# A gated feed-forward kernel whose first two iterations leave each unit's result in PSUM, with a reordered head

## The chip, the cores and the metric

The kernel runs on one NeuronCore of a Trainium2 chip. The metric is device time in microseconds (us), the median of the timed executions. The engines are TensorE (PE in the profile), VectorE (DVE), ScalarE (ACT), GpSimd (POOL) and SyncE (SP), which here only issues DMAs.

## The reference

Tokens 8192 (2 x 4096), model width 192, hidden width 2048; all data is fp32.

```python
def _attn_ref(x, weight_gen) -> np.ndarray:
...
    w = np.exp(w)
    w = w / (np.sum(w, axis=-1, keepdims=True) + 1e-09)
    pad = K - 1
    x_pad = np.concatenate([np.zeros((B, pad, D), dtype=np.float32), x], axis=1)
    idx = np.arange(S)[:, None] + np.arange(K)[None, :]
    x_unf = x_pad[:, idx, :]
    x_unf = x_unf.reshape(B, S, K, H, group)
    out = np.einsum('bshk,bskhg->bshg', w, x_unf)
...
def _moe_ref(x, w_in, w_out):
    h = x @ w_in
    g = h * np.cos(h)
    return (g @ w_out).astype(np.float32)
...
def _moe2_ref(x, w_in, w_out):
    h = x @ w_in
    g = np.maximum(0.01 * h, h)
    return (g @ w_out).astype(np.float32)
...
    x = _moe_ref(x=x, **moe_kwargs)
    return _moe2_ref(x=x, **moe2_kwargs)
```

There are 8 heads (`H`) and 7 taps (`K`).

## The kernel before

The tokens are cut into 16 chunks (`C`) of 512 (`N`), four from each of 128 partitions. For each chunk there are three parts: the window attention (`attention`, 11 instructions on VectorE: seven multiplications called taps, and four additions, into `prods`), the first network, and the second. Every fp32 product is made of products of high and low parts (`_hi`, `_lo`), since the matmuls take fp32r.

A network's 2048 hidden columns are eight **units** of two 128-column tiles. A unit goes: TensorE fills a PSUM **slot** (two banks, `slots[step % 3]`, three slots) with h; then VectorE and ScalarE form the gated value; ScalarE rounds it to `g_hi` (`high_part`, line 548), and VectorE subtracts to get `g_lo` (`pending_low`, line 710); then TensorE sums `g_hi` and `g_lo` times the output weights into the banks `acc_a` and `acc_b`. In the first network the gated value takes four instructions: `whole` (ACT, 603), the fraction (DVE, 774), the sine (ACT, 639) and the product (DVE, 788). In the second it is one Prelu (ACT, 607). In both, the result goes to the SBUF buffer `gate`, which has two halves, `q % 2`, as `g_hi` and `g_lo` have.

One **iteration** i has 18 steps. Steps 0 to 7 are units q = 0 to 7 (first network, chunk i). Steps 8, 9, 10, 11, 12, 14, 15, 17 are q = 8 to 15 (second network, chunk i - 1). Step 13 transposes an output (from iteration 2 on) and step 16 the next input, also through a slot; in iteration 0 the input has step 8. Everything is written out by hand: each engine has its own list and waits on counting semaphores. TensorE runs `both_products(i, q, j, r)`: five pairs of matmuls that begin filling unit q's slot, then the sum of unit r = q - 3 mixed with the rest of the filling.

Three rules set the order around the change.

- `wait_for_slot`: before a fill, the slot's last use must be over. Before, that is `g_ready` (a first unit's product is written to `gate`) or `leaky_ready` (its Prelu is).
- `high_part` waits for `summed` up to unit s - 2, because `g_hi` has two halves.
- `step_of` on ScalarE: at each step first the pending `g_hi` of the step before, then the sine, then the first read of the next step's slot (`first_read`: `whole` or Prelu). On VectorE: fraction, pending `g_lo`, product, then attention instructions by the table `ATT_AT` and softmax pieces by `SOFT_START` and `SOFT_END`.

The head (iterations -1 and 0) loads everything, does the softmax of the first chunks, the attention of chunk 0 on VectorE, splits the weights of the first network into high and low parts (ACT high, POOL low), and shares the attention of chunk 1 between VectorE (two taps and the last two additions) and GpSimd (seven instructions in the middle). Meanwhile TensorE runs matmuls without use (`raise_clock`). The weights of the second network are split by GpSimd in iteration 0 and 1.

## Time and profile before

| | us |
|---|---|
| median of 3 timed runs | 1177.25 |
| lowest, highest | 1176.35, 1177.26 |
| the profiled execution, its own time | 1180.46 |
| its span, first to last instruction | 1178.7 |
| TensorE busy in it | 1151.8 (98%) |
| VectorE, ScalarE, GpSimd busy | 905.8, 738.6, 94.8 |

TensorE is busy nearly throughout, so the time is the matmuls' own, plus the stretches in which TensorE waits, plus what a lowered clock costs. The chain that ended last is 90% TensorE.

### The profile page before, as it was taken

Reading aid. Unit: us, or ns where it says so; the run is one execution under the profiler, and the core shown is the slowest. Engines: PE = TensorE matmul, PEld = TensorE weight load, DVE = VectorE, ACT = ScalarE, POOL = GpSimd, SP = SyncE. Lnnn points to the kernel's source line nnn. Section 1 sums busy time; section 2 is a strip of 40 time slices with the busy share of each in tenths; the row PEclk is TensorE's granted clock in tenths of the full one; section 3 lists DMA queues with packets and bytes.
Section 4 is the critical chain, followed back from the end, with each engine's and each line's share of the span. In section 5 each row is a group of like instructions: output and inputs, shape, how many; then the busy total and the mean of one; then the engine's idle time right before and its main releaser. Section 6 shows DMA issues by size and latency. Waiting matters only on the chain.

```text
span 1178.7 us, 23306 instructions
## 1 busy us (share of the span) xinstructions
PE 1151.8 (98%) x10180; PEld 960.2 (81%) x10180; DVE 905.8 (77%) x857; ACT 738.6 (63%) x809; POOL 94.8 (8%) x87
## 2 busy tenths in 40 slices
PE   7879999999999999999999999999999999999998
PEld 5658888887878888888888888888888888888876
DVE  7778798787987869688686978868698786968533
ACT  5657675766847657575665756557575665757544
POOL 4764000000000000000000000000000000000000
PEclk9879999999999999999999999999999999999999
DMA  9400101001010010100001010010101001000000
GB/s 268 144 2 1 34 1 37 12 1 48 1 46 3 1 48 2 48 1 17 32 2 48 2 48 1 1 48 1 48 1 48 2 1 48 1 14 1 9 7 28
DMA packets 15277, 32.68 MB, mean 28 GB/s; under 512 B 5068, under 2 KB 9546, under 8 KB 14920
## 3 DMA queue, kind: packets, MB, share of 16 engines
q1 hardware_dynamic: 15176, 31.19, 8.4%
q8 instruction: 81, 1.33, 0.5%
q14 instruction: 20, 0.16, 0.0%
HBM read 24.89 MB, written 6.29 MB: 26 GB/s over the span
## 4 chain that ended last, share of the span: by engine, by line
PE 90%; DVE 4%; ACT 2%; POOL 2%; issue 1%; ACTq 0%; DVEq 0%; POOLq 0%
PE slot L940 41%; PE acc_a L940 27%; PE acc_b L940 18%; DVE g_lo L710 1%; PE slot L1136 1%; POOL prods L282 1%; DVE gate L774 1%; POOL prods L288 1%; PE acc_b L913 0%; DVE prods L282 0%; PE slot L885 0%; ACT gate L607 0%; ACT L656 0%; ACT whole L603 0%; PE slot L872 0%
## 5 line engine op out<-in xcount | busy, mean ns | idle before, releaser
L940 PE MATMUL acc_a<-g_hi,out_hi_lo 64*128 64x512 f32 x2000 | 698.9, 389 | 0.0
L710 DVE TENSOR_TENSOR g_lo<-gate,g_hi 128x1024 fp32r<-128x1024 f32 x256 | 319.7, 1249 | 115.8 <-ACT g_hi L548 115.2
L940 PEld LDWEIGHTS acc_a<-g_hi,out_hi_lo 64*128 64x128 f32 x2000 | 369.6, 185 | 36.0
L940 PE MATMUL acc_b<-g_hi,out_hi_lo 64*128 64x512 f32 x1000 | 389.8, 390 | 8.9 <-DVE g_lo L710 7.5
L940 PE MATMUL acc_a<-g_lo,out_hi_lo 64*128 64x512 f32 x1000 | 388.1, 388 | 0.0
L940 PE MATMUL acc_b<-g_lo,out_hi_lo 64*128 64x512 f32 x1000 | 387.8, 388 | 0.0
L548 ACT ACTIVATE g_hi<-gate 128x1024 fp32r<-128x1024 f32 x256 | 271.4, 1060 | 104.4 <-PE acc_b L940 82.9
L940 PE MATMUL slot<-x_a_hi,in_a_lo 64*128 64x512 f32 x1024 | 300.8, 395 | 1.6 <-DVE gate L788 1.3
L940 PE MATMUL slot<-x_a_hi,in_a_hi 64*128 64x512 f32 x1024 | 297.2, 388 | 0.0
L940 PE MATMUL slot<-x_a_lo,in_a_hi 64*128 64x512 f32 x1024 | 297.1, 388 | 0.0
L940 PE MATMUL slot<-x_b,in_b_hi 64*128 64x512 f32 x1024 | 296.9, 387 | 0.2 <-DVE x_b L724 0.2
L607 ACT ACTIVATE gate<-slot 128x1024 f32<-128x1024 f32 x128 | 130.9, 1023 | 130.0 <-PE slot L940 94.9
L940 PEld LDWEIGHTS acc_b<-g_hi,out_hi_lo 64*128 64x128 f32 x1000 | 184.8, 185 | 33.8 <-DVE g_lo L710 9.8
L940 PEld LDWEIGHTS acc_a<-g_lo,out_hi_lo 64*128 64x128 f32 x1000 | 185.0, 185 | 17.8
L940 PEld LDWEIGHTS acc_b<-g_lo,out_hi_lo 64*128 64x128 f32 x1000 | 185.0, 185 | 16.4
L774 DVE SCALAR_TENSOR_TENSOR gate<-slot,whole 128x1024 f32<-128x1024 f32 x128 | 156.2, 1220 | 50.3 <-ACT whole L603 49.6
L603 ACT ACTIVATE whole<-slot 128x1024 int32<-128x1024 f32 x128 | 131.0, 1023 | 69.3 <-PE slot L940 69.3
L788 DVE SCALAR_TENSOR_TENSOR gate<-slot,gate 128x1024 f32<-128x1024 f32 x128 | 156.4, 1222 | 6.7 <-ACT gate L639 5.0
L940 PEld LDWEIGHTS slot<-x_a_hi,in_a_lo 64*128 64x128 f32 x1024 | 143.0, 185 | 22.5 <-PE slot L940 2.9
L639 ACT ACTIVATE gate<-gate 128x1024 f32<-128x1024 f32 x128 | 135.5, 1058 | 35.8 <-DVE gate L774 33.2
L940 PEld LDWEIGHTS slot<-x_b,in_b_hi 64*128 64x128 f32 x1024 | 142.5, 185 | 18.9 <-DVE x_b L724 0.5
L940 PEld LDWEIGHTS slot<-x_a_lo,in_a_hi 64*128 64x128 f32 x1024 | 142.5, 185 | 18.6 <-DVE x_a_lo L721 0.2
(87 smaller groups left out, 1058.0 us busy)
## 6 DMA issues: line engine op xcount, KB each, us to landing
x_win<-in_x SPq DMA_DIRECT2D x14, 960.0 KB, 4.7
out<-result SPq DMA_DIRECT2D x16, 384.0 KB, 2.4
out_raw<-in_moe_w_out SPq DMA_DIRECT2D x2, 1024.0 KB, 14.1
taps_w<-in_weight_gen SPq DMA_DIRECT2D x2, 560.0 KB, 8.2
out_raw<-in_moe_w_out SPq DMA_DIRECT2D x2, 512.0 KB, 11.0
in_a_raw<-in_moe_w_in SPq DMA_DIRECT2D x1, 1024.0 KB, 9.0
in_b_raw<-in_moe_w_in SPq DMA_DIRECT2D x2, 512.0 KB, 10.8
in_a_raw<-in_moe_w_in SPq DMA_DIRECT2D x2, 384.0 KB, 6.3
```

The lines of the kernel that those rows point to most:

```text
L282: engine.tensor_tensor(prods[:, to, :].rearrange("p (r g) -> p r g", g=group), view[:, k * heads:(k + J) * heads, :], w.unsqueeze(2).to_br ...
L288: engine.tensor_tensor(prods[:, to, :], prods[:, a, :], prods[:, b, :], ALU.add).then_inc(att, 1)
L548: nc.scalar.activation(g_hi[:, q % 2, :], gate[:, q % 2, :], ACT.Copy)\
L603: nc.scalar.activation(whole[:, q % 2, :], slot, ACT.Identity, bias=0.25)\
L607: nc.scalar.activation(gate[:, q % 2, :], slot, ACT.Prelu, alpha=0.01)\
L639: nc.scalar.activation(gate[:, q % 2, :], gate[:, q % 2, :], ACT.Sin, scale=TURN).then_inc(cos_ready, 1)
L710: nc.vector.tensor_tensor(g_lo[:, q % 2, :], gate[:, q % 2, :], g_hi[:, q % 2, :].bitcast(FP32), ALU.subtract)\
L774: nc.vector.scalar_tensor_tensor(gate[:, q % 2, :], slot, 0.25, whole[:, q % 2, :], ALU.add, ALU.subtract)\
L788: nc.vector.scalar_tensor_tensor(gate[:, q % 2, :], slot, RADIANS, gate[:, q % 2, :], ALU.mult, ALU.mult)\
L940: return nc.tensor.matmul(to, w[rows, :], x[rows, :], start=start, stop=stop)
L1136: nc.tensor.matmul(slots[LAG - 1][:, 0, :], g_hi[:, 0, N + k % 2 * P:N + (k % 2 + 1) * P], g_hi[:, 0, 0:N], start=True, stop=True)
```

## The change

Four things are changed together.

1. **Results stay in the slots** in iterations 0 and 1 (`stays`, `result_of`): the product or the Prelu is written back over the slot, and `g_hi` and `g_lo` are made from the slot instead of `gate`. `wait_for_slot` then waits for `lo_ready` of the slot's unit in place of `g_ready` or `leaky_ready`.
2. **The first unit in halves**: unit 0's six steps between fill and sum are twelve instructions of 512 columns, with semaphores `unit_act` and `unit_dve`.
3. **The head**: softmax chunks are (0,1), (1,3), ... in place of (0,2), (2,3), ...; the softmax product of the second and the two VectorE taps of chunk 1 move behind units 1, 2 and 3; the output weights of the first network load in two halves and ahead of chunk 1's window; ScalarE makes their high parts one step later; GpSimd does two taps of chunk 1 between the first and the second piece of their low parts; the last two additions of chunk 1 come after step 6, not 5 (`ATT_END`); at step 7 the split of the next input comes behind the pending `g_hi` and `g_lo`.
4. **Later softmax pieces** are moved: the three exponentials (two table loads each) from (1,13), (2,16), (3,16) to (1,10), (3,10), (5,10), and their beginnings and ends with them.

```diff
+    def stays(i):
+
+
+        return i <= 1
...
-        ATT_DVE, ATT_POOL, ATT_END = 2, 9, 5
+        ATT_DVE, ATT_POOL, ATT_END = 2, 9, 6
...
-        SOFT_CHUNKS = [(0, 2), (2, 3), (3, 6), (6, 11), (11, C)]
+        SOFT_CHUNKS = [(0, 1), (1, 3), (3, 6), (6, 11), (11, C)]
...
-        SOFT_START, EXP_AT, SOFT_END = [[(1, 9), (2, 14), (3, 14)], [(1, 13), (2, 16), (3, 16)],
-                                        [(1, 15), (3, 9), (4, 9)]]
+        SOFT_START, EXP_AT, SOFT_END = [[(1, 8), (2, 13), (4, 13)], [(1, 10), (3, 10), (5, 10)],
+                                        [(1, 13), (3, 13), (5, 13)]]
...
+        def result_of(i, q):
+
+            if stays(i):
+                return slots[UNITS[q] % SLOTS][:, :, :].rearrange("p a n -> p (a n)")
+            return gate[:, q % 2, :]
...
+            load_gen(0)
+            load_own(0)
+            load_halo(0)
+            load_columns(0)
+            load_gen(1)
+            load_columns(1)
+            load_columns(2)
+            load_out(W1, w_out1, slice(0, TILES // 2), out_loaded[0])
+            load_out(W1, w_out1, slice(TILES // 2, TILES), out_loaded[1])
+            load_own(1)
+            load_halo(1)
...
+            for n in range(len(LO_PIECES)):
+                column_lows(n)
+            out_lows(0)
...
-            pool.wait_ge(att, ATT_STEPS + ATT_DVE)
-            for instruction in list(attention(1, pool))[ATT_DVE:ATT_POOL]:
+            of_pool = list(attention(1, pool))[ATT_DVE:ATT_POOL]
+            for instruction in of_pool[:2]:
+                instruction()
+            for n in range(1, len(OUT_PIECES)):
+                out_lows(n)
+            for instruction in of_pool[2:]:
                 instruction()
...
             def high_part(i, q):
                 s = unit(i, q)
+                if s == 0:
+                    act.wait_ge(unit_dve, 2)
+                    nc.scalar.activation(g_hi[:, 0, 0:N], slots[0][:, 0, :], ACT.Copy)\
+                        .then_inc(unit_act, 1)
+                    act.wait_ge(g_ready, 1)
+                    nc.scalar.activation(g_hi[:, 0, N:], slots[0][:, 1, :], ACT.Copy)\
+                        .then_inc(hi_ready, 1)
+                    return
...
-                nc.scalar.activation(g_hi[:, q % 2, :], gate[:, q % 2, :], ACT.Copy)\
+                nc.scalar.activation(g_hi[:, q % 2, :], result_of(i, q), ACT.Copy)\
                     .then_inc(hi_ready, 1)
...
-                    nc.scalar.activation(gate[:, q % 2, :], slot, ACT.Prelu, alpha=0.01)\
+                    nc.scalar.activation(result_of(i, q), slot, ACT.Prelu, alpha=0.01)\
                         .then_inc(leaky_ready, 1)
...
-                    nc.vector.tensor_tensor(g_lo[:, q % 2, :], gate[:, q % 2, :],
+                    nc.vector.tensor_tensor(g_lo[:, q % 2, :], result_of(i - b, q),
                                             g_hi[:, q % 2, :].bitcast(FP32), ALU.subtract)\
                         .then_inc(lo_ready, 1)
...
-                    nc.vector.scalar_tensor_tensor(gate[:, q % 2, :], slot, RADIANS,
+                    nc.vector.scalar_tensor_tensor(result_of(i, q), slot, RADIANS,
                                                    gate[:, q % 2, :], ALU.mult, ALU.mult)\
                         .then_inc(g_ready, 1)
...
-            softmax_end(1)
-
-            first_two = list(attention(1, dve))
-            first_two[0]()
+            softmax_inverse_sum(1)
+
+            of_chunk_1 = list(attention(1, dve))
             for step in range(STEPS):
                 step_of(0, step)
-                if 0 < step < ATT_DVE:
-                    first_two[step]()
+                if step == 1:
+                    softmax_multiply(1)
+                if 1 < step <= ATT_DVE + 1:
+                    of_chunk_1[step - 2]()
                 if step == ATT_END:
-                    for instruction in first_two[ATT_POOL:]:
+                    for instruction in of_chunk_1[ATT_POOL:]:
                         instruction()
...
                 j, s = used[-1]
                 what = kind(j, s)
-                if what == "first":
+                if what in ("first", "second") and stays(j):
+                    if unit(j, UNITS.index(s)) == 0:
+                        pe.wait_ge(unit_dve, 3)
+                    pe.wait_ge(lo_ready, unit(j, UNITS.index(s)) + 1)
+                elif what == "first":
                     pe.wait_ge(g_ready, first_units(j, UNITS.index(s)))
                 elif what == "second":
                     pe.wait_ge(leaky_ready, second_units(j, UNITS.index(s)))
```

How the instructions stand, at three places. In these rows `slot0` to `slot2` are the three slots and `[waits ...]` names the semaphores that an instruction waits for.

TensorE, iteration 1: the first matmul that fills unit 13 (step 14), unit 14 (step 15), unit 15 (step 17), and unit 0 of iteration 2. Before:

```order
L940 MATMUL slot2<-x2_a_hi,in2_a_lo 128x512 [waits leaky_ready]
...
L940 MATMUL slot0<-x2_a_hi,in2_a_lo 128x512 [waits leaky_ready]
...
L940 MATMUL acc_a<-g_hi,out2_hi_lo 128x512 [waits att,leaky_ready]
...
L940 MATMUL slot0<-x1_a_hi,in1_a_lo 128x512 [waits x1_hi,leaky_ready]
```

Now (the same places in the list; the third is the wait ahead of the input transposes):

```order
L1055 MATMUL slot2<-x2_a_hi,in2_a_lo 128x512 [waits lo_ready]
...
L1055 MATMUL slot0<-x2_a_hi,in2_a_lo 128x512 [waits lo_ready]
...
L1055 MATMUL acc_a<-g_hi,out2_hi_lo 128x512 [waits att,lo_ready]
...
L1055 MATMUL slot0<-x1_a_hi,in1_a_lo 128x512 [waits x1_hi,lo_ready]
```

What moved is the semaphore, from the Prelu of the slot's unit to its `g_lo`; the matmuls stand as they stood.

ScalarE, iteration 1, from the Prelu of unit 11 to the Prelu of unit 14. Before (the first row is unit 11's Prelu):

```order
L607 ACTIVATE gate<-slot2 128x1024 [waits lo_ready,filled]
L548 ACTIVATE g_hi<-gate 128x1024 [waits summed,leaky_ready]
L607 ACTIVATE gate<-slot0 128x1024 [waits lo_ready,filled]
L548 ACTIVATE g_hi<-gate 128x1024 [waits summed,leaky_ready] x2
L607 ACTIVATE gate<-slot2 128x1024 [waits lo_ready,filled]
L661 ACT_TABLE_LOAD
L661 ACTIVATE taps_w<-taps_w 128x672 [waits soft]
L656 ACT_TABLE_LOAD
L656 ACTIVATE spare<-ident 1x1
L607 ACTIVATE gate<-slot0 128x1024 [waits lo_ready,filled]
```

Now:

```order
L671 ACTIVATE slot2<-slot2 128x1024 [waits lo_ready,filled]
L732 ACT_TABLE_LOAD
L732 ACTIVATE taps_w<-taps_w 128x672 [waits soft]
L727 ACT_TABLE_LOAD
L727 ACTIVATE spare<-ident 1x1
L607 ACTIVATE g_hi<-slot1 128x1024 [waits summed,leaky_ready]
L671 ACTIVATE slot0<-slot0 128x1024 [waits lo_ready,filled]
L607 ACTIVATE g_hi<-slot2 128x1024 [waits summed,leaky_ready]
L607 ACTIVATE g_hi<-slot0 128x1024 [waits summed,leaky_ready]
L671 ACTIVATE slot2<-slot2 128x1024 [waits lo_ready,filled]
L671 ACTIVATE slot0<-slot0 128x1024 [waits lo_ready,filled]
```

The exponential with its two table loads moved from behind unit 13's Prelu to ahead of unit 10's `g_hi`.

GpSimd in the head: the low parts of the output weights (`out1_hi_lo`, four pieces of two instructions) and its share of chunk 1's attention (`prods`). Before, from the last piece on:

```order
L484 TENSOR_TENSOR out1_hi_lo<-out1_raw,out1_hi_lo 128x4x64 [waits w1_hi]
L484 TENSOR_TENSOR out1_hi_lo<-out1_raw,out1_hi_lo 128x4x128
L282 TENSOR_TENSOR prods<-x_win1,taps_w 128x768 [waits att]
L282 TENSOR_TENSOR prods<-x_win1,taps_w 128x768
L288 TENSOR_TENSOR prods<-prods 128x1536 [waits att]
```

Now, from the second instruction of the first piece to the end of the second:

```order
L525 TENSOR_TENSOR out1_hi_lo<-out1_raw,out1_hi_lo 128x4x128
L297 TENSOR_TENSOR prods<-x_win1,taps_w 128x768 [waits filled,x_zeroed,att,halo1_loaded,own1_loaded,soft]
L297 TENSOR_TENSOR prods<-x_win1,taps_w 128x768
L525 TENSOR_TENSOR out1_hi_lo<-out1_raw,out1_hi_lo 128x4x64 [waits w1_out_hi]
L525 TENSOR_TENSOR out1_hi_lo<-out1_raw,out1_hi_lo 128x4x128
```

Two of the taps moved from behind the fourth piece to behind the first.

## Rows read from the trace of the kernel before

**Rows 1.** The page: busy time of each engine, and one group of instructions.

```profile
PE 1151.8 (98%) x10180; PEld 960.2 (81%) x10180; DVE 905.8 (77%) x857; ACT 738.6 (63%) x809; POOL 94.8 (8%) x87
...
L788 DVE SCALAR_TENSOR_TENSOR gate<-slot,gate 128x1024 f32<-128x1024 f32 x128 | 156.4, 1222 | 6.7 <-ACT gate L639 5.0
```

**Rows 2.** Timeline of PE: start, duration, instruction, count, idle before and releaser.

```profile
34.78 0.79 PE L940 MATMUL acc_b<-g_hi,out_hi_lo 64*128 64x512 f32 x1 [2.19 <-DVE g_lo L710]
...
63.14 0.37 PE L872 MATMUL slot<-ident,prods 64*128 64x64 f32 x2 [4.86 <-DVE prods L288]
...
65.31 0.80 PE L913 MATMUL acc_b<-g_hi,out_hi_lo 128*128 128x512 f32 x1 [1.06 <-DVE g_lo L710]
...
85.60 0.79 PE L940 MATMUL acc_b<-g_hi,out_hi_lo 64*128 64x512 f32 x1 [2.50 <-DVE g_lo L710]
```

**Rows 3.** Windows: stretch, length, five engines' busy time, clock, DMA share, GB/s.

```profile
28.00:32.00 4.00, 2.68 (x22) 1.57 (x22) 2.87 (x3) 3.20 (x5) 2.76 (x4) 1.00 0.99 230
...
64.00:68.00 4.00, 2.94 (x12) 2.16 (x8) 3.32 (x5) 3.79 (x6) 0.00 (x0) 0.50 0.02 6
68.00:72.00 4.00, 4.00 (x17) 2.73 (x17) 3.97 (x4) 1.89 (x2) 1.03 (x1) 0.56 0.00 0
...
84.00:88.00 4.00, 2.40 (x12) 1.91 (x14) 4.00 (x4) 1.58 (x3) 3.92 (x5) 0.65 0.01 4
```

**Rows 4.** Timeline of POOL in the head.

```profile
41.38 2.00 POOL L484 TENSOR_TENSOR out_hi_lo<-out_raw,out_hi_lo 128x256 fp32r<-128x256 f32 x2 [3.38 <-ACT out_hi_lo L686]
43.34 4.04 POOL L282 TENSOR_TENSOR prods<-x_win,taps_w 128x768 f32<-128x768 f32 x2
47.45 4.39 POOL L288 TENSOR_TENSOR prods<-prods 128x1536 f32<-128x1536 f32 x1
...
55.92 3.47 POOL L288 TENSOR_TENSOR prods<-prods 128x1536 f32<-128x1536 f32 x1
59.47 1.54 POOL L282 TENSOR_TENSOR prods<-x_win,taps_w 128x768 f32<-128x768 f32 x1
```

**Rows 5.** Timeline of DVE, iteration 1.

```profile
82.37 3.18 DVE L710 TENSOR_TENSOR g_lo<-gate,g_hi 128x1024 fp32r<-128x1024 f32 x1
...
124.81 1.75 DVE L288 TENSOR_TENSOR prods<-prods 128x1536 f32<-128x1536 f32 x1
126.59 0.96 DVE L282 TENSOR_TENSOR prods<-x_win,taps_w 128x768 f32<-128x768 f32 x1
127.47 1.22 DVE L710 TENSOR_TENSOR g_lo<-gate,g_hi 128x1024 fp32r<-128x1024 f32 x1
```

**Rows 6.** Timeline of PE, first matmuls of units 12, 14, 15 and of iteration 2.

```profile
124.81 0.40 PE L940 MATMUL slot<-x_a_hi,in_a_lo 64*128 64x512 f32 x2
...
133.43 0.39 PE L940 MATMUL slot<-x_a_hi,in_a_lo 64*128 64x512 f32 x2
...
138.18 0.47 PE L940 MATMUL slot<-x_a_hi,in_a_lo 64*128 64x512 f32 x2
...
142.62 0.39 PE L940 MATMUL slot<-x_a_hi,in_a_lo 64*128 64x512 f32 x2
```

**Rows 7.** Timeline of ACT, iteration 1, steps 10 to 16.

```profile
124.98 1.03 ACT L607 ACTIVATE gate<-slot 128x1024 f32<-128x1024 f32 x1 [1.90 <-DVE g_lo L710]
...
133.70 1.07 ACT L548 ACTIVATE g_hi<-gate 128x1024 fp32r<-128x1024 f32 x1 [2.94 <-PE acc_b L940]
...
135.69 1.28 ACT L661 ACT_TABLE_LOAD   x1
...
139.17 1.00 ACT L607 ACTIVATE gate<-slot 128x1024 f32<-128x1024 f32 x1
140.08 0.57 ACT L560 ACTIVATE x_a_hi<-slot 128x512 fp32r<-128x512 f32 x1
...
141.81 2.13 ACT L548 ACTIVATE g_hi<-gate 128x1024 fp32r<-128x1024 f32 x2
```

**Rows 8.** Waits of PE from 160 to 1100 us: us, times, longest.

```profile
PE acc_b L940 <- DVE g_lo L710: 2.5, 2, 1.3
PE acc_b L940 <- DVE res_b L745: 1.4, 2, 0.7
```

More of the change, by code:

```diff
@@ L222, in window_attention_two_ffn @@
         in_loaded = [sem(f"in{n}_loaded") for n in range(3)]
-        out_loaded = sem("out_loaded")
+        out_loaded = [sem(f"out{n}_loaded") for n in range(2)]
         w2_loaded = [sem(f"w2_{n}_loaded") for n in ("a", "b", "out")]
@@ L309, in rest_of_window, with third, start @@
                     engine.wait_ge(halo_loaded[c], 64)
+            def third():
+                if c == 1:
+                    wait_for_chunk()
+                    wait_for_halo()
+                tap(4, 2)
+            def start():
+                wait_for_chunk()
+                tap(6, 0)
+            def rest_of_window():
+                wait_for_halo()
                 tap(5, 1)
@@ L599, in first_read @@
                 slot = slots[step % SLOTS][:, :, :].rearrange("p a n -> p (a n)")
+                if unit(i, q) == 0:
+                    for cols, done in ((slice(0, N), unit_act), (slice(N, None), whole_ready)):
+                        nc.scalar.activation(whole[:, 0, cols], slot[:, cols], ACT.Identity, bias=0.25)\
+                            .then_inc(done, 1)
+                    return
                 if step in FIRST_UNITS:
@@ new lines, in column_turns, with column_highs_b @@
+            def column_turns(n):
+                cols = HI_PIECES[n]
+                a_raw = W1.in_a_raw[:, cols]
+                nc.scalar.activation(a_raw, a_raw, ACT.Copy, scale=PER_TURN).then_inc(w1_hi, 1)
+                nc.scalar.activation(b_lows(W1.in_b_lo_raw, cols), b_pairs(W1.in_b_raw, cols), ACT.Copy,
+                                     scale=PER_TURN).then_inc(w1_raw, 1)
+            def column_highs_b(n):
+                cols = HI_PIECES[n]
+                act.wait_ge(w1_raw, n + 1)
+                both = slice(cols.start + (P if n else 0), cols.stop + P)
+                nc.scalar.activation(W1.in_b_hi[:, both], W1.in_b_raw[:, both], ACT.Copy, scale=PER_TURN)\
+                    .then_inc(w1_hi, 1)
@@ L682, in _ @@
             load_sine()
-            act.wait_ge(out_loaded, 32)
-            def out_high(n):
-                for high, _, raw in out_parts(W1, OUT_PIECES[n]):
-                    nc.scalar.activation(high, raw, ACT.Copy).then_inc(w1_hi, 1)
-            out_high(0)
-            first_read(-1, STEPS - 1)
-            for i in range(LAST):
+            first_read(-1, STEPS - 1)
+            for step in range(STEPS):
+                step_of(0, step)
+                if step < len(OUT_PIECES):
+                    out_high(step)
+            for i in range(1, LAST):
                 for step in range(STEPS):
                     step_of(i, step)
-                    if i == 0 and step + 1 < len(OUT_PIECES):
-                        out_high(step + 1)
             for step in range(STEPS + LAG):
@@ L766, in step_of @@
                     split_low(INPUT_STEP, i + 1)
-                if step == FIRST_INPUT_SPLIT and input_splits(i, step):
-                    split_low(FIRST_INPUT_STEP, i + 1)
-                if in_first:
+                if in_first and i == 0 and step == FIRST_UNITS[0]:
+                    q = 0
+                    for cols, ready, n, done in ((slice(0, N), unit_act, 1, unit_dve),
+                                                 (slice(N, None), whole_ready, 1, fraction)):
+                        dve.wait_ge(ready, n)
+                        nc.vector.scalar_tensor_tensor(gate[:, 0, cols], slot[:, cols], 0.25,
+                                                       whole[:, 0, cols], ALU.add, ALU.subtract)\
+                            .then_inc(done, 1)
+                elif in_first:
                     q = UNITS.index(step)
@@ L777, in step_of @@
                 pending_low(i, step)
+                if step == FIRST_INPUT_SPLIT and input_splits(i, step):
+                    split_low(FIRST_INPUT_STEP, i + 1)
                 j = first_out(i, step)
```

133 lines of the change are left out of this document (84 added, 49 removed).

## The prediction

> **What bounds the kernel now.** I read four views, in this order. The page's busy times say who sets the end: TensorE, at 1151.8 of 1178.7 us [rows 1]. So an edit counts only by the time it takes from, or gives to, TensorE's waits and its clock. The timeline of PE says where it waits: nearly all of its idle time lies ahead of 90 us. The reader should see four places in it: 2.19 us at 34.78, 4.86 at 63.14, 1.06 at 65.31 and 2.50 at 85.60 [rows 2]. The windows show the clock: at 1.00 from 28 to 32, though TensorE was idle for 1.3 us in it, but at 0.50 and 0.56 in the 8 us after the 4.86 wait, and 0.65 in the 4 us after the 2.50 one [rows 3]. Full clock is 2.4 GHz and 0.50 is 1.2 GHz. Last, the timelines of ACT and DVE in the second half of iteration 1 show the path from a filled slot to its g_lo [rows 5, 7]. From 90 to 142 us TensorE never waits, and later only for 3.9 us in four places [rows 8]. Whatever delays it there goes to the end one for one.
>
> **A unit's pitch.** Unit 12 of iteration 1 begins at 124.81 and unit 14 at 133.43, so a unit takes (133.43 - 124.81) / 2 = 4.31 us [rows 6]. A fill of unit q takes the slot of three steps before. Where the steps are all units, that is unit q - 3, whose g_lo TensorE needs 1.1 us later anyway, for the sum. There the new wait on lo_ready costs at most 1.1 us where g_lo was late already, and nothing else.
>
> **What the head gives.** Four terms, all against TensorE's idle places.
>
> 1. GpSimd's share of chunk 1 sets the 4.86 wait. It runs from 43.34 to 61.0 in five groups of the timeline (first to last [rows 4]). Now its first two taps (4.04) go ahead of the second low piece, into time in which GpSimd waited for ScalarE (3.38 us ahead of the last piece alone [rows 4], and two shorter waits). That takes 4.0 off what stands behind the last piece. In addition VectorE's g_lo no longer reads two SBUF operands while GpSimd works. The addition took 4.39 beside VectorE and 3.47 when VectorE was idle: 0.9 less, and as much again for the two middle taps by the ratio 3.47/4.39. Sum 5.8 us: the transposes at 63.14 come at about 57.3. The rest of the new head (half units, smaller first softmax) makes TensorE reach this place earlier, and wait there; I count it at nothing. Should GpSimd turn out faster, this cover is gone and the head is worth up to 2 more. Should ScalarE's later high parts hold GpSimd up, it is worth up to 2 less.
> 2. The 1.06 wait at 65.31 was for unit 5's g_lo, which stood behind the last two additions. These now come after step 6, so it is done earlier: 1.1 us.
> 3. The 2.50 wait at 85.60. The g_lo there took 3.18 beside GpSimd's weight work [rows 5]; reading a slot it should take 1.22, as the products do that read one PSUM and one SBUF operand, mean 1222 ns over 128 [rows 1]. So 2.0 less, but the fill that ran before the wait now stands behind it (1.1): 0.9.
> 4. The wait left there is then about 1.9, between the 1.3 that kept the clock and the 2.50 that lost it, 0.35 x 4 = 1.4 us [rows 3]. I take half, 0.7.
>
> Together 8.5 us, between 5 and 11. On term 3, the row shows that g_lo stretches beside GpSimd and the product does not. The Trainium skill (SBUF — State Buffer, Who interferes with whom) says that a VectorE instruction with two SBUF inputs contends with a GpSimd instruction that reads SBUF, and one with at most one does not. By it the term stands; were it wrong and g_lo stayed at 3.18, the sum would be 2.0 us worse.
>
> **The moved softmax pieces after iteration 1.** The two g_lo waits (2.5) and two res_b waits (1.4) [rows 8] stand next to the old ends at (3,9), (4,9) and the old exponentials at (2,16), (3,16), and go. The two new exponentials at (3,10), (5,10) hold ScalarE for a good 3.5 us (139.17 - 135.69 [rows 7]) ahead of a g_hi that is summed two units on. No row shows that place; the nearest are those four waits, 0.7 to 1.3 each, and a gain cannot come of a block. I take 1.1 each, 2.2. Net gain 1.7, bounds 1.3 and 2.5.
>
> **What the slots cost in iteration 1.** Steps 13 and 16 are no units, so behind them the distance shrinks: step 14 takes the slot of step 11, that is unit 13 that of unit 11; unit 14 that of 12; unit 15 that of 13; and unit 0 of iteration 2 that of 14. That is two units, not three. Before, a fill needed only the Prelu of the slot's unit. Now it needs its g_lo, which needs its g_hi, which waits for `summed` of the unit two before. That sum is the very one that TensorE ends just before this fill: the row at 133.70 shows g_hi of unit 12 released by PE at the end of unit 13 [rows 7]. So at each of the four places TensorE stands for at least g_hi 1.07 + g_lo 1.22 [rows 5, 7], with 0.1 of semaphores: 2.4 us. Place by place, on the clock of the trace before:
>
> - **Unit 13** (before at 124.81 + 4.31 = 129.12). ScalarE now has the exponential here. Unit 11's Prelu began at 124.98, held by unit 9's g_lo, which now comes 0.7 earlier without the softmax beginning ahead of it: the Prelu ends at 125.3. Then 3.5 of exponential, g_hi(10) 1.05, g_lo(10) 1.2: 131.1. Then VectorE has its addition and tap, 1.75 + 0.96 [rows 5], while ScalarE makes Prelu 12 and g_hi(11); then g_lo(11) 1.2: 135.0. Delay 5.9 us.
> - **Unit 14**: + 2.4, total 8.3.
> - **Unit 15**: its slot's g_hi stands behind the input's split on ScalarE, 141.81 - 140.08 = 1.73 [rows 7], which starts 0.3 us after TensorE is through with the transposes. So 0.3 + 1.73 + 1.07 + 1.22 = 4.3. Total 12.6.
> - **Unit 0 of iteration 2** (before at 142.62 [rows 6]): + 2.4, total 15.0. The softmax end that stood here is gone and gave TensorE a 0.3 us wait; 14.7 is left.
>
> The clock comes on top. After 2.50 idle the loss was 1.4 us; after 4.86 it was 0.50 x 4 + 0.44 x 4 = 3.8 [rows 3]. For the waits of 5.9, 4.3, 2.4 and 2.4 us I take 3.8, 2.6 (between), 1.4 and 1.4, in all 9.2. The lower bound is 0; the upper is the low clock through all four units, 4 x 4.31 = 17.2.
>
> **Sum** against the profiled execution: 1180.46 - 8.5 - 1.7 + 14.7 + 9.2 = 1194.2. It stands 3.2 above the median 1177.25, so by the median 1177.25 + 13.7 = **1191.0 us**.
>
> **The rivals.**
>
> - **The stalls come, the clock holds.** For it: 1.3 us idle in 28 to 32 left it at 1.00. Against: both waits of over 2 us in rows 2 that stand alone lost it. Clock cost 2 in place of 9.2: 1177.25 - 10.2 + 14.7 + 2 = 1183.8.
> - **The clock stays low through the four units**, since each new wait comes 4 to 8 us after the last: 1177.25 - 10.2 + 14.7 + 17.2 = 1199.0.
> - **The slot wait is covered, and it is faster.** The place is unit 13's fill. If g_lo(11) is done by the end of unit 12, and likewise 12, 13, 14, the wait costs nothing and the head's gain stands: 1177.25 - 8.5 - 1.7 = 1167.0. It decides at 4.31 us after unit 12's start. Against it: g_hi(12) ran at 133.70, after unit 13's last matmul, with ScalarE idle for 2.94 us ahead of it [rows 7]; it could not run earlier, so g_lo(12) cannot.
> - **The edits cancel.** The exponential costs less at unit 13 than I think (stall 2.4 there, 3.5 less), the clock falls little and the head gives 11 or more: within 2 us of 1177.
>
> **How the numbers follow.** A difference of 0.2%, 2.4 us, is about what a measurement of this kernel can tell from none. Chances: forecast (1185 to 1197) 0.52; clock holds (1179.6 to 1185) 0.20; clock stays low (above 1197) 0.12; cancel, within 0.2%, 0.09; faster 0.07. So slower 0.84, same 0.09, faster 0.07. The range 1179 to 1198 leaves out the faster case, nearly all of the cancelling one and about half of the low-clock one, 0.2 in all.
>
> **What would show it.** In the changed kernel's timeline of PE: transposes of chunk 1 near 57; g_lo at 1.2 us while GpSimd is busy; four idle places named after g_lo ahead of units 13, 14, 15 and unit 0 of iteration 2, of about 5.9, 2.4, 4.3 and 2.4 us, in a stretch of some 30 us that took 18; and windows with a clock under 1.00 between them. I am wrong if those four places are missing, if the clock stands at 1.00 through them, or if the head's waits went down by less than 5 us.

## The result, and the profile after

The changed kernel takes **1190.42 us** (median of 4 runs, 1189.70 to 1191.91) against 1177.17 for the kernel before: ratio 1.0104, interval 1.0083 to 1.0125. It is slower by 13.3 us; the forecast was 13.7. In a second series of runs it took 1189.57 (ratio 1.0100, 1.0082 to 1.0118). The profiled execution took 1189.70, span 1187.9; before, 1180.46 and 1178.7. So the traces differ by only 9.2, 4 us less than the medians: the first trace of before stood 3.3 above its median, that of after 0.7 below. The second trace of the kernel before, further down, shows what most of the 3.3 is.

The first view of the kernel after is the waits of PE over the whole span: instruction that waited, what released it, us in total, times, longest.

```profile
PE slot L1055 <- DVE g_lo L803: 16.4, 5, 5.8
...
PE slot L987 <- DVE prods L303: 4.6, 1, 4.6
PE acc_b L1055 <- DVE g_lo L803: 2.6, 4, 0.8
PE slot L1055 <- DVE g_lo L794: 1.5, 1, 1.5
```

Before, no fill ever waited for a g_lo. Now six do (the destination is slot and the releaser g_lo): five with 16.4 us together, and one with 1.5 (L794, unit 0's halves), where the kernel before had a wait of 1.25 for a product. The timeline of PE places the five; L1055 is the matmuls of `both_products`, L987 the transposes of chunk 1, and the number in brackets is the idle time ahead.

```profile
58.41 0.28 PE L987 MATMUL slot<-ident,prods 64*128 64x64 f32 x2 [4.56 <-DVE prods L303]
...
76.08 0.50 PE L1055 MATMUL slot<-x_a_hi,in_a_lo 64*128 64x512 f32 x2 [1.64 <-DVE g_lo L803]
...
115.01 0.40 PE L1055 MATMUL slot<-x_a_hi,in_a_lo 64*128 64x512 f32 x2
...
125.27 0.80 PE L1055 MATMUL slot<-x_a_hi,in_a_lo 64*128 64x512 f32 x2 [5.78 <-DVE g_lo L803]
...
134.78 0.51 PE L1055 MATMUL slot<-x_a_hi,in_a_lo 64*128 64x512 f32 x2 [2.44 <-DVE g_lo L803]
...
144.03 0.62 PE L1055 MATMUL slot<-x_a_hi,in_a_lo 64*128 64x512 f32 x2 [4.13 <-DVE g_lo L803]
...
152.68 0.51 PE L1055 MATMUL slot<-x_a_hi,in_a_lo 64*128 64x512 f32 x2 [2.44 <-DVE g_lo L803]
```

Read it in three steps. Unit 12 begins at 115.01 where it began at 124.81 [rows 6]: by then the new head has gained 9.8 us. The last four rows are the first matmuls of units 13, 14, 15 and of unit 0 of iteration 2. Iteration 2 begins at 152.68 where it began at 142.62 [rows 6]: 10.1 late. So a stretch that took 17.8 us took 37.7: 19.9 more, which eats the 9.8 and leaves 10.1 of loss. Later 0.9 of it comes back.

The timelines of ACT and DVE say why each of the last four waits is at least 2.4 long.

```profile
132.45 1.02 ACT L607 ACTIVATE g_hi<-slot 128x1024 fp32r<-128x1024 f32 x1 [9.00 <-PE acc_b L1055]
...
150.35 1.02 ACT L607 ACTIVATE g_hi<-slot 128x1024 fp32r<-128x1024 f32 x1 [7.63 <-PE acc_b L1055]
```

```profile
133.50 1.23 DVE L803 TENSOR_TENSOR g_lo<-slot,g_hi 128x1024 fp32r<-128x1024 f32 x1 [5.44 <-ACT g_hi L607]
...
151.40 1.23 DVE L803 TENSOR_TENSOR g_lo<-slot,g_hi 128x1024 fp32r<-128x1024 f32 x1 [7.43 <-ACT g_hi L607]
```

ScalarE had been idle for 9.00 us, and what released g_hi is PE's sum into acc_b. TensorE ends a sum at 132.34 (134.78 - 2.44), g_hi starts at 132.45, g_lo at 133.50, TensorE goes on at 134.78. A ring of three engines, each waiting for the one before it, with nothing else running.

The clock: windows of 4 us with stretch, length, PE's busy time (and instructions), granted clock, DMA share and GB/s.

```profile
120.00:124.00 4.00, 0.00 (x0) 0.97 0.00 0
124.00:128.00 4.00, 2.73 (x14) 0.50 0.26 48
128.00:132.00 4.00, 4.00 (x28) 0.67 0.49 202
132.00:136.00 4.00, 1.56 (x14) 1.00 0.00 0
136.00:140.00 4.00, 3.90 (x46) 1.00 0.00 0
140.00:144.00 4.00, 0.00 (x0) 1.00 0.00 0
144.00:148.00 4.00, 3.97 (x20) 0.57 0.00 0
148.00:152.00 4.00, 2.24 (x20) 1.00 0.00 0
152.00:156.00 4.00, 3.32 (x28) 1.00 0.01 4
```

The clock fell to its low level (0.50) behind the waits of 5.78 and 4.13, not behind the two of 2.44. Loss: 0.50 x 4 + 0.33 x 4 + 0.43 x 4 = 5.0 us, of which some 0.6 fell into the waits themselves. With 14.8 of waits that is 19.2 to 19.8 of the 19.9. The forecast had 9.2 for the clock.

### The profile page after: what moved, and what is told of

It reads as the page before. It is cut to its first block, busy times and chain, and to the rows that moved or that the text cites. A ratio compares the mean times of both kernels' runs of the same rounds, so it can differ in the third digit from the quotient of the medians.

```text
span 1187.9 us, 23318 instructions
## 1 busy us (share of the span) xinstructions
PE 1152.2 (97%) x10180; PEld 1020.2 (86%) x10180; DVE 897.1 (76%) x860; ACT 737.9 (62%) x812; POOL 85.7 (7%) x87
## 4 chain that ended last, share of the span: by engine, by line
PE 89%; DVE 5%; ACT 3%; POOL 2%; issue 1%; ACTq 0%; POOLq 0%; DVEq 0%
PE slot L1055 41%; PE acc_a L1055 27%; PE acc_b L1055 18%; DVE g_lo L803 2%; PE slot L1257 1%; DVE prods L303 1%; ACT g_hi L607 1%; POOL prods L303 1%; DVE prods L297 0%; POOL prods L297 0%; PE acc_b L1028 0%; ACT L727 0%; ACT L732 0%; PE slot L987 0%; PE slot L1000 0%
## 5 line engine op out<-in xcount | busy, mean ns | idle before, releaser
L1055 PE MATMUL acc_a<-g_hi,out_hi_lo 64*128 64x512 f32 x2000 | 698.0, 389 | 0.0
L1055 PE MATMUL acc_b<-g_hi,out_hi_lo 64*128 64x512 f32 x1000 | 389.6, 390 | 2.6 <-DVE g_lo L803 2.6
L1055 PEld LDWEIGHTS acc_a<-g_hi,out_hi_lo 64*128 64x128 f32 x2000 | 368.8, 184 | 24.7 <-issue 0.5
L1055 PE MATMUL acc_b<-g_lo,out_hi_lo 64*128 64x512 f32 x1000 | 387.5, 387 | 0.0
L1055 PE MATMUL acc_a<-g_lo,out_hi_lo 64*128 64x512 f32 x1000 | 387.2, 387 | 0.0
L803 DVE TENSOR_TENSOR g_lo<-gate,g_hi 128x1024 fp32r<-128x1024 f32 x232 | 283.1, 1221 | 116.6 <-ACT g_hi L607 116.2
L1055 PE MATMUL slot<-x_a_hi,in_a_lo 64*128 64x512 f32 x1024 | 305.1, 396 | 18.3 <-DVE g_lo L803 16.4
L607 ACT ACTIVATE g_hi<-gate 128x1024 fp32r<-128x1024 f32 x232 | 245.9, 1060 | 90.6 <-PE acc_b L1055 77.6
L1055 PE MATMUL slot<-x_b,in_b_hi 64*128 64x512 f32 x1024 | 300.9, 388 | 0.2 <-DVE x_b L817 0.2
L1055 PE MATMUL slot<-x_a_lo,in_a_hi 64*128 64x512 f32 x1024 | 301.0, 388 | 0.0
L1055 PE MATMUL slot<-x_a_hi,in_a_hi 64*128 64x512 f32 x1024 | 300.9, 388 | 0.0
L1055 PEld LDWEIGHTS acc_b<-g_hi,out_hi_lo 64*128 64x128 f32 x1000 | 184.6, 185 | 20.6 <-issue 5.6
L671 ACT ACTIVATE gate<-slot 128x1024 f32<-128x1024 f32 x120 | 122.6, 1022 | 119.4 <-PE slot L1055 89.5
L1055 PEld LDWEIGHTS acc_a<-g_lo,out_hi_lo 64*128 64x128 f32 x1000 | 184.7, 185 | 10.7
L1055 PEld LDWEIGHTS acc_b<-g_lo,out_hi_lo 64*128 64x128 f32 x1000 | 184.7, 185 | 10.4
L1055 PEld LDWEIGHTS slot<-x_a_hi,in_a_lo 64*128 64x128 f32 x1024 | 146.4, 185 | 34.8 <-DVE g_lo L803 18.7
L1055 PEld LDWEIGHTS slot<-x_b,in_b_hi 64*128 64x128 f32 x1024 | 146.3, 185 | 12.3 <-DVE x_b L817 0.5
L1055 PEld LDWEIGHTS slot<-x_a_lo,in_a_hi 64*128 64x128 f32 x1024 | 146.3, 185 | 12.1 <-DVE x_a_lo L814 0.2
L1055 PEld LDWEIGHTS slot<-x_a_hi,in_a_hi 64*128 64x128 f32 x1024 | 146.4, 185 | 10.1
```

The lines of the kernel that those rows point to most:

```text
L607: nc.scalar.activation(g_hi[:, q % 2, :], result_of(i, q), ACT.Copy)\
L671: nc.scalar.activation(result_of(i, q), slot, ACT.Prelu, alpha=0.01)\
L803: nc.vector.tensor_tensor(g_lo[:, q % 2, :], result_of(i - b, q), g_hi[:, q % 2, :].bitcast(FP32), ALU.subtract)\
L1055: return nc.tensor.matmul(to, w[rows, :], x[rows, :], start=start, stop=stop)
```

## The experiments

"Kernel e1" and so on are short for the labels below. Ratios are against the kernel before, run beside each on the same chip.

### Slots in iteration 0 alone (e1)

```diff
     def stays(i):
-        return i <= 1
+        return i == 0
```

> The changed kernel, but results stay in their slots in iteration 0 alone; iteration 1 writes them to gate again. My theory (the two-unit lag behind steps 13 and 16 is what costs): all four waits for g_lo at the fills of units 13, 14, 15 and of unit 0 of iteration 2 are gone (14.5 us net), and so is the low clock behind two of them (about 5 us); the head keeps its gain. By the profiled executions iteration 2 then begins at about 133 us (142.62 before, 152.68 after) and the time is 1166 to 1171 us. Rival 1 (the slots of iteration 1 carry part of the gain, since g_lo reads PSUM there): 1171 to 1176. Rival 2 (the loss is from the moved exponentials and softmax ends, not from the slots): 1184 us or more, with waits of 2 us or more left between 115 and 145 us.

Measured: **1169.62 us, ratio 0.9934 (0.9919 to 0.9950)**. Faster than both kernels, and no form below can be told from it as faster still. The waits of PE between 100 and 160 us are down to one line, and that one waits for a sum, not for a fill:

```profile
PE acc_b L1055 <- DVE g_lo L803: 0.9, 1, 0.9
```

Unit 12 begins within 0.3 us of where the changed kernel has it (114.78), iteration 2 at 133.95, 18.7 earlier than 152.68, with the clock at 1.00 between. So the slots of iteration 1 cost about 20 us (1190.42 - 1169.62 = 20.8 by the medians, 19.0 by the spans), and the rest of the change gives 7.2 by the medians of this series (1176.82 - 1169.62) and 9.8 by the spans (1178.7 - 1168.9, with the trace of before that stood 3.3 above its median). By the ratios the slots of iteration 1 cost 20.0. The expected range of 1166 to 1171 held it; rival 2 falls.

### One network's slots at a time in iteration 1 (e2 and e10)

```diff
-    def stays(i):
-        return i <= 1
+    def stays(i, q):                                  # e2
+        return i == 0 or (i == 1 and q < 8)
+    def stays(i, q):                                  # e10
+        return i == 0 or (i == 1 and q >= 8)
```

> As the kernel with slots in iteration 0 alone, but in iteration 1 the first network's eight units (steps 0 to 7) stay in their slots too, the second network's eight do not. Of the four late fills each takes the slot of a second-network unit, so by my theory (only fills two units behind are late) none of the four waits comes back: within 2 us of the kernel with iteration 0 alone, 1166 to 1171 us. Rival (waiting for g_lo costs wherever the results stay, three units apart too, since g_lo follows g_hi behind other work): at least 3 us above that kernel, with waits for g_lo at fills between 76 and 115 us.

> The changed kernel, where in iteration 1 only the second network's eight units stay in their slots (the first network's write to gate). The complement of the kernel with the first network's alone, which had none of the four waits. My theory: the whole loss of iteration 1 is here, four waits for g_lo of 5.8, 2.4, 4.1 and 2.4 us at the fills of units 13, 14, 15 and of unit 0 of iteration 2 (unit 14's slot belongs to the second network), and the time is that of the changed kernel, 1190.4, within 2 us. Rival (the first network's slots carry part of the loss): 1187 us or less.

Measured: e2 1170.89 (0.9945, 0.9929 to 0.9960); e10 **1189.49** (1.0093, 1.0077 to 1.0109). Waits of PE, 100 to 160 us, of e2:

```profile
PE acc_b L1055 <- DVE g_lo L803: 0.9, 1, 0.9
```

and of e10:

```profile
PE slot L1055 <- DVE g_lo L803: 14.8, 4, 5.8
```

Nearly the whole loss lies with the second network's units. That alone could be the network (Prelu in place of a sine) as well as the lag. But behind units 11 to 14 one of steps 13 and 16 lies, so that the fill that takes their slot comes two units later and not three, and in e10 exactly the four fills of these slots wait. The fills of units 11 and 12, three units behind second-network units that also stay in their slots, do not wait at all. So it is the lag. The first network's slots may not be quite free. Their kernel stands 1.3 us above e1, which this measurement hardly tells from 0, but its trace has a wait of 1.67 for a fill at 76.64, where e1 and e10 wait 0.5 for a sum. That is the "at most 1.1" of the prediction, for a fill that now stands behind a late g_lo.

### The schedule or the softmax pieces: slots in iterations 0 to 15 (e5)

```diff
-        return i <= 1
+        return i < LAST
```

> The changed kernel, with results in slots in iterations 0 to 15. If the cost is the schedule's (two-unit lag behind steps 13 and 16), it recurs in each of the 14 further iterations: 2.4 at unit 13 (no exponential), 2.4, 4.1 and 2.4 us, in all 11.3, plus 1.7 of clock behind the 4.1 one: 14 x 13.0 = 182, so 1372 us. If the clock also falls behind each 2.4 us wait (1.4 each): 14 x 17.2 = 241, so 1431. Rival (the stalls are iteration 1's own, by the softmax pieces there): under 1230 us.

Measured: 1416.09 (1.2039, 1.2010 to 1.2068), 225.7 more than the changed kernel, 16.1 in each of 14 further iterations. Iteration 4 stands for the others (timeline of PE):

```profile
389.82 0.50 PE L1055 MATMUL slot<-x_a_hi,in_a_lo 64*128 64x512 f32 x2 [2.23 <-DVE g_lo L803]
...
396.86 0.50 PE L1055 MATMUL slot<-x_a_hi,in_a_lo 64*128 64x512 f32 x2 [2.44 <-DVE g_lo L803]
...
405.80 0.79 PE L1055 MATMUL slot<-x_a_hi,in_a_lo 64*128 64x512 f32 x2 [3.86 <-DVE g_lo L803]
...
414.28 0.50 PE L1055 MATMUL slot<-x_a_hi,in_a_lo 64*128 64x512 f32 x2 [2.44 <-DVE g_lo L803]
```

The time lies between the two that were expected, 1372 and 1431. Without softmax pieces the four waits stay, 11.0 us in all, so they are the schedule's. Of the other 5.1 of each iteration some 3.9 are clock, by what follows. Part of the rest is an extra wait in iterations 3 and 5, which have an exponential at step 10, for a sum: 3.27 us at 298.48 and 3.25 at 474.92. What the remainder is was not settled. This kernel is also the best place to look at the clock, since its one trace repeats the same waits at many moments. They are not independent draws: iterations 4, 7, 8, 11 and 14 have the same four outcomes (kept, kept, lost, lost). Behind 30 waits of 2.43 or 2.44 us the granted clock of the next 6 us was 1.00 in 15 cases, and fell in the other 15, costing 1.5 to 1.7 us each. Behind 11 waits of 2.23 or 2.24 it fell four times, for 1.7. Behind the 13 of 3.86 or 3.87 it fell each time, for 1.4 to 1.7. (1.6 + 2 x 0.85 + 0.6 = 3.9 for an iteration.) One of each of the first kind, in windows of 2 us (the waits end at 311.29 and 328.82):

```profile
311.00:313.00 2.00, 1.71 (x14) 1.00 0.02 4
313.00:315.00 2.00, 2.00 (x20) 1.00 0.00 0
315.00:317.00 2.00, 1.37 (x24) 1.00 0.00 0
328.50:330.50 2.00, 1.68 (x14) 0.97 0.04 8
330.50:332.50 2.00, 2.00 (x12) 0.50 0.00 0
332.50:334.50 2.00, 2.00 (x16) 0.68 0.00 0
```

### The exponential moved out of iteration 1 (e4)

```diff
-        SOFT_START, EXP_AT, SOFT_END = [[(1, 8), (2, 13), (4, 13)], [(1, 10), (3, 10), (5, 10)],
-                                        [(1, 13), (3, 13), (5, 13)]]
+        SOFT_START, EXP_AT, SOFT_END = [[(1, 8), (2, 13), (4, 13)], [(2, 2), (3, 10), (5, 10)],
+                                        [(2, 4), (3, 13), (5, 13)]]
```

> The changed kernel, with the third chunk's exponential at step 2 of iteration 2 instead of step 10 of iteration 1, and its softmax end at step 4 of iteration 2. My theory: unit 13's wait of 5.8 us holds 3.4 of exponential and goes to about 2.4; the other three stay 2.4, 4.1 and 2.4. The clock, which fell behind 5.8 and not behind 2.4, then holds there, 3.3 us more. At steps 2 and 4 of iteration 2 every unit has three units of lag: no wait, or one of at most 1.3. So 1190.4 - 3.4 - 3.3 = 1183.7, between 1183 and 1187. Rival 1 (the exponential only filled time in which ScalarE waited for sums anyway): unit 13's wait stays above 5 us and the time within 1 us of 1190. Rival 2 (a shorter wait loses the clock as well): 1187.

Measured: 1188.92 (1.0105, 1.0085 to 1.0125), 1.5 us below the changed kernel by the medians, nothing by the ratios, where 6.7 had been expected. The waits of PE, 100 to 200 us:

```profile
PE slot L1055 <- DVE g_lo L803: 11.7, 4, 4.1
PE acc_b L1055 <- DVE g_lo L803: 2.7, 2, 1.6
```

The first half of the expectation came true: unit 13's wait is 2.69, so the exponential had held 3.1 us of it (rival 1 falls). But at its new place the exponential costs 2.7 us of waits for sums, where I had expected none or 1.3. And in this trace the clock gave nothing back, though it is the trace of the slowest of six executions, 1192.86, 3.9 above the median. By the medians the clock gave back 1.1 us at most (1.5 less the 0.4 that the waits differ by), not the 3.3 that I had expected. In the trace it fell behind 2.69, 4.14 and this time behind the last 2.44, whose like kept it in the changed kernel, and also behind a wait of 1.67 at 76.04. A wait of 2.7 us in place of 5.8 is no guarantee that the clock holds.

### What in the head pays (e3 and e8)

Both start from e1. e3 keeps the slots for the first unit alone:

```diff
-    def stays(i):
-        return i == 0
+    def stays(i, q):
+        return i == 0 and q == 0
```

> Slots kept for the first unit of iteration 0 alone (its halves need it); units 1 to 7 write to gate again, so their g_lo reads two SBUF operands beside GpSimd. Measured against the kernel with slots in all of iteration 0 (1169.6 us). My theory (terms 1, 3 and 4 of the prediction's head): g_lo during GpSimd's weight work is back at about 3.2 us instead of 1.22 and the wait for it at about 76 us is 2.5 instead of 1.6 or less, 0.9 to 2.6 us with the clock; GpSimd's additions slow down, and the transposes of chunk 1 come 0.9 to 1.8 us later than 58.2. In all 171.4 to 174 us above 1000: 1171.4 to 1174. Rival (the slots bring nothing in the head, only its new order does): within 1 us of 1169.6.

e8 puts GpSimd's first two taps back behind the low parts:

```diff
-            for instruction in of_pool[:2]:
-                instruction()
             for n in range(1, len(OUT_PIECES)):
                 out_lows(n)
-            for instruction in of_pool[2:]:
+            for instruction in of_pool:
                 instruction()
```

> Slots in iteration 0 alone, with GpSimd's first two taps of chunk 1 back behind the last three groups of second low parts. My theory (term 1, 4.0 of 5.8 us): the order of GpSimd's work sets the wait at the transposes; they come 2.2 us later (the idle 1.75 and 0.92 us ahead of the taps and the last pair return to it as waiting, at most 3 us later), at 60.4 to 61.2 instead of 58.14, and the time is 1171.5 to 1173. Rival (VectorE's later end of the attention, at step 6 instead of 5, sets the transposes): unmoved within 0.3 us, time within 1 us of 1169.6.

Measured: e3 **1174.52** (0.9973, 0.9962 to 0.9984), e8 **1173.79** (0.9961, 0.9947 to 0.9975). Both medians lie 0.5 to 0.8 us above the expected ranges. Against e1's 0.9934 the ratios give 4.6 and 3.2 us. In both, the wait ahead of chunk 1's transposes is 7.5 us where e1 has 4.57. In e3 TensorE had also waited 0.94 us for a g_lo before that, at 46.09. Counted from TensorE's first wait in the head (31.53 in e1, 30.75 in e3, 30.80 in e8), the transposes come 4.2 us later than e1's in e3 and 2.7 later in e8. From e3, in this order, PE, POOL and DVE:

```profile
61.55 0.37 PE L987 MATMUL slot<-ident,prods 64*128 64x64 f32 x2 [7.53 <-DVE prods L303]
```

```profile
53.51 4.30 POOL L303 TENSOR_TENSOR prods<-prods 128x1536 f32<-128x1536 f32 x1
```

```profile
68.33 3.45 DVE L803 TENSOR_TENSOR g_lo<-gate,g_hi 128x1024 fp32r<-128x1024 f32 x1 [1.55 <-ACT g_hi L607]
```

e1's addition on GpSimd that answers to the second row:

```profile
50.89 3.49 POOL L303 TENSOR_TENSOR prods<-prods 128x1536 f32<-128x1536 f32 x1
```

With g_lo from gate both engines stretch: the addition from 3.49 to 4.30, a g_lo from 1.23 to 3.45. So the slots of iteration 0 pay 4 to 5 us, more than the 1.8 in term 1 plus the 0.9 in term 3 that I gave them. The order of the taps pays about 3, where term 1 had 4.0. No run takes back the half units, the smaller first softmax or the order of the loads by themselves.

### The softmax pieces alone (e7)

e1 with all later softmax pieces where the kernel before has them:

```diff
-        SOFT_START, EXP_AT, SOFT_END = [[(1, 8), (2, 13), (4, 13)], [(1, 10), (3, 10), (5, 10)],
-                                        [(1, 13), (3, 13), (5, 13)]]
+        SOFT_START, EXP_AT, SOFT_END = [[(1, 9), (2, 14), (3, 14)], [(1, 13), (2, 16), (3, 16)],
+                                        [(1, 15), (3, 9), (4, 9)]]
```

> Slots in iteration 0 alone, and the softmax pieces of chunks 3 to 15 where the kernel before has them. Theory: the moved pieces gave about 0.7 us (waits behind 115 us: 3.5 us in the kernel with slots in iteration 0 alone, 4.2 in the kernel before), so 1170.3. The prediction had 1.7: 1171.3. Rival (the move cost): 1168.6 or less.

Measured: 1171.17 (0.9937, 0.9923 to 0.9951), 0.3 us above e1 by the ratios. That agrees with 0.7, but this measurement cannot tell 0.7 from 0 or from 1.7. The waits behind 115 us do: those of its trace are the 0.3, 2.5 and 1.4 of the kernel before, those of e1 are 0.9 and 2.6. That is 0.7 less waiting.

### One more tap for VectorE (e11)

```diff
-        ATT_DVE, ATT_POOL, ATT_END = 2, 9, 6
+        ATT_DVE, ATT_POOL, ATT_END = 2, 8, 6
```

> Slots in iteration 0 alone, and the last tap of chunk 1 that GpSimd made (1.54 us, with VectorE idle for 2.99 us behind it) is made by VectorE (0.95). Theory: the transposes come 0.6 us earlier than 58.14 and everything after them too: 0.9926 of the kernel before, 0.6 us below the kernel with slots in iteration 0 alone, which is within the measurement. Rival (VectorE then starts the addition later): no change or worse.

Measured: 1169.77 (0.9925, 0.9908 to 0.9941): not to be told from e1. That the ratio is nearly the expected 0.9926 is luck, as the waits show. Waits of PE in its head:

```profile
PE slot L987 <- DVE prods L303: 3.9, 1, 3.9
PE acc_b L1055 <- DVE g_lo L803: 1.6, 1, 1.6
```

The wait at the transposes went from 4.6 to 3.9 as expected, but a wait of 0.5 behind it (at 76.97 in e1) became 1.6. It was for this g_lo, in the timeline of DVE, whose like takes 1.23 in e1:

```profile
73.82 2.33 DVE L803 TENSOR_TENSOR g_lo<-gate,g_hi 128x1024 fp32r<-128x1024 f32 x1
```

GpSimd had begun a pair of subtractions at 73.09 (1.98 us in all), and this g_lo came in behind it; in e1 the g_lo began at 75.69, between two of GpSimd's. What was gained at one wait was given back at the next. The last section tells why.

### The kernel before and the changed kernel, once more

> The kernel before, once more, for a second trace. My theory: the waits are the same in every execution (2.2 at 34.8, 4.9 at 63.1, 1.1, 2.5 at 85.6), but which of the waits of about 2.5 us lose the clock differs from one to the next, and explains that the first profiled execution stood 3.2 us above the median. Expected: the same waits within 0.3 us, a time of 1176 to 1178 us, and a granted clock above 0.50 in at least one of the windows that had 0.50 to 0.75 before (32:40, 64:72, 84:88). Rival (the 3.2 us lie outside TensorE's stretch): clocks as in the first trace.

Measured: 1177.9 us in a single execution, span 1176.1 (first trace 1178.7). The theory was wrong in a useful way: it is not only the clock that differs, a wait does. The waits of PE between 60 and 100 us of this second trace:

```profile
PE slot L872 <- DVE prods L288: 4.8, 1, 4.8
PE acc_b L913 <- DVE g_lo L710: 1.1, 1, 1.1
PE acc_b L940 <- DVE g_lo L710: 0.9, 2, 0.5
```

The wait of 2.50 at 85.60 [rows 2] is one of 0.54 here, and the clock behind it stays at 1.00:

```profile
83.84 0.49 PE L940 MATMUL acc_b<-g_hi,out_hi_lo 64*128 64x512 f32 x1 [0.54 <-DVE g_lo L710]
```

That is 2.0 us less waiting and some 1.4 less of low clock. The low spell behind the transposes is shorter too (68:72 at 0.90 where the first trace has 0.56), with the same waits of 4.8 and 1.06 ahead of it. Against this stand a new wait of 0.40 and a start 0.6 later, so that the spans differ by 2.6. Unit 12 begins at 121.67 here and at 124.81 in the first trace.

> The changed kernel once more, for a second trace and on the same chip as the other two. Theory: the same waits within 0.3 us; the two waits of 2.44 us lose the clock in some executions and not in others, 1.7 us each, so the profiled execution's low windows lie elsewhere than in the first trace, or fewer or more; ratio 1.011 (1.008 to 1.014). Rival (the clock follows the length of the wait alone): the same windows at the same clock within 0.05.

Measured: 1189.57 (1.0100, 1.0082 to 1.0118). The same four waits, 14.8 us, and here the rival was right: in windows of 2 us from the end of each wait the clock was 0.50, 0.50, 0.67 behind the first, 0.56, 0.59, 1.00 behind the third and 1.00 behind the two of 2.44, all within 0.01 of the first trace. Unit 12 begins at 115.67 and iteration 2 at 153.34, so the stretch between them took 37.7 us here as well, against 17.8 in the second trace of the kernel before (121.67 to 139.47).

## Why the prediction was right, point by point

The total was right within 0.6 us. But the two halves under it were each 3 us too big, and that they cancelled is luck: the forecast had -10.2 and +23.9; the runs show -7.2 (e1) and +20.8 (changed kernel against e1). The second traces say the same: -6.0 at unit 12, +19.9 in the stretch behind it and -0.7 by the softmax pieces make 13.2, against 13.3 measured.

**The four waits: right.** Forecast 5.9, 2.4, 4.3, 2.4; traced 5.78, 2.44, 4.13, 2.44, in two traces and again in e10. The step that carried it was to ask which step each fill takes its slot from, and what releases that unit's g_hi: [rows 7] had the answer in the kernel before. The path to the first wait went as told, too: from the Prelu of unit 11 to the end of its g_lo it took 10.6 us (114.66 to 125.22), where the forecast had 10.0 (124.98 to 135.0). Kernel e10, with four waits behind its two-unit lags and none behind the others, shows the lag to be the cause, e5 that it recurs, e4 that 3.1 us of the first was the exponential (forecast 3.5).

**The clock: mis-sized, 9.2 for 5.0.** The failed step is "For the waits of 5.9, 4.3, 2.4 and 2.4 us I take 3.8, 2.6 (between), 1.4 and 1.4". A wait of 2.44 does not cost 1.4 each time; in e5 it costs 1.5 to 1.7 in half of 30 cases and 0 in the others, 0.85 on average. One of 3.9 costs 1.4 to 1.7, not 2.6. By these prices the term would have been 2.7 + 1.7 + 0.85 + 0.85 = 6.1, where 2.7 is what the trace lost behind the 5.78 once the matmuls ran again, and 1.7 behind the 4.13. My rows were single samples. The same two windows (64:72) that cost 3.8 in the first trace, behind the waits of 4.86 and 1.06, cost 2.4 in the second, behind the same waits. And the price of the 2.50 left out the next window, 88:92 at 0.93, another 0.3. What sets the price of a wait stays open.

**The head: forecast 8.5; at unit 12 it is 9.8 between the first traces and 6.0 between the second; 7.2 with the softmax pieces by the medians.**

- Term 1 (5.8). The transposes came at 58.41 instead of 63.14, 4.7 earlier, forecast 57.3. The cover named there held: TensorE comes to the place at 53.85 instead of 58.28 and waits 4.56, so GpSimd's chain still ends last. It comes earlier since the wait of 2.19 at 34.78 is gone, and with it a low clock that cost 3.0 us in both traces of the kernel before (0.50 for 6 us). Its split was off: I gave the order 4.0 and the slots 1.8; e8 and e3 each make the wait 2.9 longer, and cost 3.2 and 4.6 us.
- Term 2 (1.1): the 1.06 wait is gone.
- Terms 3 and 4 (0.9 + 0.7). The g_lo of 3.18 now takes 1.23 beside GpSimd, the wait is 1.64, and the clock is at 1.00 behind it. (Term 4 says "about 1.9", but term 3 leaves 2.50 - 0.9 = 1.6.) But the price of a kept clock was 1.7, not 0.7, and the second trace of the kernel before shows that the 2.50 wait is not in every execution. Where it is 0.54, these terms are worth little: that is most of the difference between 9.8 and 6.0.
- Not in the sum: the clock comes back sooner after the transposes. In the first trace before it stayed at 0.50 through 64:68 and 0.56 through 68:72 [rows 3]; now 60:64 has 0.71 and 64:68 has 1.00. But the second trace before, with the 1.06 wait, has 0.90 in 68:72, so most of this is not shown to come of the change.

**The softmax pieces: 1.7 forecast, 0.7 seen.** The 3.9 us went as forecast, but 2.6 came in their place instead of 2.2, in four waits of at most 0.8, and 0.9 in iteration 1 instead of 0.3. The failed step is "No row shows that place; the nearest are those four waits": I had counted two new places, and there are five.

**The base.** "It stands 3.2 above the median" was right to use. Had I set the sum against the profiled execution alone, the forecast would have been 3.8 us too high. But the base and the terms 3 and 4 do not fit together: the second trace, near the median, has 0.54 in place of the wait of 2.50, and the sum took 1.6 off the median for that wait all the same.

**The rivals.** Clock holds: not so, though with 5.0 the truth lies between it and the forecast. Clock stays low: not so, behind the 5.78 it is back after 5.4 us, behind the 4.13 after about 3.6. Covered: refuted by the four rows. Cancel: refuted.

**The signs.** Four waits at the four places, g_lo at 1.2 and windows under 1.00: all there. Two did not fit. The stretch was to take "some 30 us", while the sum itself makes it 17.8 + 14.7 + 9.2 = 41.7, and it took 37.7. And the head's waits were to go down by 5 us or more: the four of [rows 2] make 10.6, those of the changed kernel 4.56 and 1.64, so 4.4 less. That sign was badly chosen, since TensorE arriving early at the transposes lengthens the wait there and costs nothing; when the transposes run was the thing to look at.

## What to carry to other kernels

When a buffer is to be held longer, list for every reuse how many steps lie between its last reader and its next writer, where the schedule has its exceptions above all. A lag of three units was nearly free here (at most 1.1 us, at one fill) and a lag of two cost a full pass through two other engines, 2.4 us each, since the last reader waited for the very engine that now waited for it. A change that is right for one phase (iteration 0, with GpSimd busy: worth 4 to 5 us) need not be carried into the next: limited to iteration 0, it makes the kernel 0.66% faster than before. And a second trace of the same kernel helps to tell which waits are its own and which are one execution's luck.
